# One GpSimd subtraction over a whole tile in place of seven and of four over slices of 256 columns

## The chip, the cores and the metric

The program runs on one core of a Trainium2 chip. Its time is the device time of one execution in microseconds (us); lower is better. The kernel before takes 2143.12 us, the median of 3 runs (2141.82 to 2145.76).

A core has five engines with a queue each, and they meet only at semaphores: TensorE (PE in the profile; its weight loads are PEld), VectorE (DVE), ScalarE (ACT), GpSimd (POOL) and SyncE (SP), which here issues the DMAs. An engine works through its queue in order; an instruction that waits holds up everything behind it on that engine.

## The reference, cut to what matters

Three layers follow each other: windowed attention, a mixture of eight experts with a gating matrix that is normalised eight times over rows and columns, and a feed-forward layer with a leaky activation.

```python
# attention: q, k, v are (4, 8, 576, 64); window 128, a linear bias per head
scores = np.where(mask, scale * q @ k.T + bias, -1e9)
attn = exp(scores - max); attn = attn / (sum(attn) + 1e-9)
x = (attn @ v)                                   # laid out as (2304, 512)

# experts: w1 (8, 512, 1024), w2 (8, 1024, 512)
P = np.exp(x @ w_gate - max)
for _ in range(8):
    P /= P.sum(1, keepdims=True) + 1e-09
    P /= P.sum(0, keepdims=True) + 1e-09
    P *= N / E
for e in range(E):
    out += P[:, e:e+1] * (np.maximum(x @ w1[e], 0.0) @ w2[e])

# feed-forward: w_in (512, 2048), w_out (2048, 512)
h = out @ w_in
return np.maximum(0.01 * h, h) @ w_out
```

## The kernel before, in words

**Stages.** Attention takes the first 175 us or so of the span. Then come 80 "granules": 32 of the experts for the first half of the tokens (numbers 0 to 31), 32 for the second half (32 to 63), 8 of the feed-forward layer for the first half (64 to 71) and 8 for the second (72 to 79). A granule is a slice of 256 hidden columns of one expert or of the feed-forward layer. It has two "units", u = 0 with 256 columns of tokens per operand and u = 1 with 320. Where the half or the layer changes (before granules 32, 64 and 72; a "turn" in what follows), the operands made from x are built anew.

**Weights in two parts.** To keep accuracy each operand of a matmul is held as a high part (the value rounded to the fast float type) and a low part (value minus high part), and each product is three matmuls: high x high, low x high, high x low (lines 1110, 1112 and 1113 up; 1132, 1133 and 1134 down).

**Seven products.** The up-projection of a unit is done as a two-by-two block product with seven products instead of eight. Its operands on the weight side are seven blocks of 256 columns, three raw and four sums. The weights arrive by DMA in `stage_up` (512 KB) and `stage_down` (512 KB). GpSimd makes the blocks and splits them, in `split_up`: four sums of 256 columns (lines 351 to 356), one cast of all 7 x 256 = 1792 columns to `up_hi` (line 358), then the subtraction that gives `up_lo` (line 362). `split_down` does the same for the 1024 columns of the down weights, with a cast (line 368) and a subtraction (line 372). GpSimd's last instruction of each gives the semaphore that TensorE waits for (`up_split`, `down_split`), and that lets SyncE load the next weights.

**When GpSimd works.** There are two sets of split weights. `both(n, s)` (line 436) splits the weights of granule n when TensorE has done the last up product of granule n - 2 (`a_done`), and the down weights when it has done that granule's last down product (`y_done`). So the up split of granule n runs while TensorE is in unit u = 0 of granule n - 1. Two of the 80 splits are made elsewhere: that of granule 0 during attention, and that of granule 1 at its end.

**A unit on the other engines.** TensorE's order in a unit is: two products, a tile of down-projection, two products (the second named A12 and S2 in the code), a tile, the products S4 and S3, a tile, the product A22, one or two tiles. S3 waits for ScalarE's copy `u2` (line 542), A22 waits for VectorE's sum `c22s` (line 863). VectorE's order is: the result of a tile (line 751 or 757), the sum `c11s` (857), the result of a tile, the low part of `c11s` (878), the sums `c22s` (863) and `c12s` (869), a result, the low parts of `c22s`, of `c12s` and of the last block (878), results. In the feed-forward layer the low parts are line 884, and the leaky activation adds in-place operations on `c11s`, `c22s` and `c12s` (887). ScalarE makes the high parts: after the copies of a unit's start it waits for `c11s` (line 593, or 616 in the feed-forward layer), and only then makes the copy `u2`.

The lines that read two operands in SBUF on VectorE are 878 for `c11s` and `c12s` and `c22s` (with `hs_hi`), 884 and 887, and at the turns 834 to 851; lines 857, 863, 869, 751 and 757 have one operand in PSUM.

Of the kernel before, what the change touches and what calls it, by code (L numbers as in the profile page):

```python
# [5 lines left out]
def attention_moe_ffn(nc, q, k, v, w_gate, w_up, w_down, out):  # L6
# [6 lines left out]
    ALU, ACT, AX = mybir.AluOpType, mybir.ActivationFunctionType, mybir.AxisListType  # L13
# [4 lines left out]
    D, E = w_gate.shape  # L18
# [3 lines left out]
    FG = 256  # L22
# [17 lines left out]
    OPS = 7  # L40
# [8 lines left out]
    with ctx:  # L49
# [3 lines left out]
        def place(name, cols, dt=fp32):  # L53
            t = nc.alloc_sbuf_tensor_at(name, [P, cols], dt, offset=at[0])
            at[0] += (cols + 7) // 8 * 32
            return t
# [11 lines left out]
        up_hi, up_lo, down_hi, down_lo, slot_at = [], [], [], [], []  # L68
# [7 lines left out]
        stage_up = place("stage_up", (OPS + 1) * FG)  # L76
        stage_down = place("stage_down", 2 * D)
# [50 lines left out]
        def sem(name):  # L128
            return ctx.enter_context(nc.semaphore(name))
# [19 lines left out]
        up_ready, down_ready, w_step, up_split, down_split = (  # L149
            sem(n) for n in ("up_ready", "down_ready", "w_step", "up_split", "down_split"))  # L150
# [173 lines left out]
        def _(pool):  # L324
            g = nc.gpsimd
# [16 lines left out]
            def raw(op):  # L342
                return stage_up[:, (op + 1) * FG:(op + 2) * FG]
# [3 lines left out]
            def split_up(n, s):  # L347

                pool.wait_ge(up_ready, 16 * (n + 1))
                base = 5 * n  # L350
                g.tensor_tensor(raw(T1), b12, raw(B11), ALU.subtract).then_inc(w_step, 1)  # L351
                g.tensor_tensor(raw(T3), raw(B22), b12, ALU.subtract)
                pool.wait_ge(w_step, base + 1)
                g.tensor_tensor(raw(T2), raw(B22), raw(T1), ALU.subtract).then_inc(w_step, 1)
                pool.wait_ge(w_step, base + 2)
                g.tensor_tensor(raw(T4), raw(B21), raw(T2), ALU.subtract).then_inc(w_step, 1)
                pool.wait_ge(w_step, base + 3)
                g.tensor_copy(up_hi[s][:, :], stage_up[:, FG:]).then_inc(w_step, 1)  # L358
                pool.wait_ge(w_step, base + 4)
                for op in range(OPS):  # L360
                    part = slice(op * FG, (op + 1) * FG)
                    last = g.tensor_tensor(up_lo[s][:, part], raw(op), up_hi[s][:, part], ALU.subtract)  # L362
                last.then_inc(up_split, 1)

            def split_down(n, s):

                pool.wait_ge(down_ready, 16 * (n + 1))
                g.tensor_copy(down_hi[s][:, :], stage_down[:, :]).then_inc(w_step, 1)  # L368
                pool.wait_ge(w_step, 5 * n + 5)
                for c in range(0, 2 * D, FG):  # L370
                    part = slice(c, c + FG)
                    last = g.tensor_tensor(down_lo[s][:, part], stage_down[:, part], down_hi[s][:, part], ALU.subtract)  # L372
                last.then_inc(down_split, 1)

            split_up(0, 0)
            split_down(0, 0)

            def first_operands(u):
# [43 lines left out]

            pool.wait_ge(p_tr, GROUPS * ITERS)
            split_up(1, 1)
            split_down(1, 1)

            def raw_lows(phase, u):
# [8 lines left out]
            def both(n, s):  # L436

                pool.wait_ge(a_done, 4 * 2 * (n - 1))
                split_up(n, s)
                pool.wait_ge(y_done, TILES * (n - 1))  # L440
                split_down(n, s)
# [861 lines left out]
```

## Time and profile before

| | |
|---|---|
| runs, median (lowest to highest) | 2143.12 us (2141.82 to 2145.76) |
| profiled execution, its own time | 2145.76 us |
| profiled execution, span of the core | 2142.8 us |
| TensorE busy | 2094.1 us, 98% of the span |
| VectorE busy | 1299.9 us, 61% |
| GpSimd busy | 1212.8 us, 57% |
| ScalarE busy | 627.7 us, 29% |
| chain of waits, by engine | PE 88%, DVE 9%, issue 3% |
| mean granted TensorE clock | 0.983 of full |

The span is what the instructions of the program cover; the execution's own time is some 3 us more. A busy share near 100% says which engine the others have to feed. The share of an engine that is not the bound counts only where the bound waits for it. The rows further down give a start in us from the span's start, a duration, the engine, the line of the kernel, the operation, what it writes and reads, and the shape.

### The profile page before, as it was taken

The page shows a single profiled execution, that of the slowest core. Times are in us where ns is not written, and L with a number is a line of the kernel's source. Part 1 is how long each engine was busy: PE and PEld are TensorE (multiplying, and loading weights), DVE is VectorE, ACT ScalarE, POOL GpSimd, SP SyncE. Part 2 cuts the span into 40 slices and gives each one's busy share as a digit, 9 for nine tenths or more (in the row PEclk, how much of TensorE's full clock was granted, in tenths as well). Part 3 has the DMA queues.
Part 4 walks back from the last instruction along what each step waited for, and adds up shares of the span by engine and source line. Part 5 has one row for each costly group of instructions (what it writes and reads, how often), then busy time and mean ns, then how long its engine had stood idle before and what let it go on. Part 6 is the DMA issues. An engine that isn't in the chain of part 4 may idle for free.

```text
span 2142.8 us, 37354 instructions
## 1 busy us (share of the span) xinstructions
PE 2094.1 (98%) x12635; PEld 1857.9 (87%) x12635; DVE 1299.9 (61%) x2743; ACT 627.7 (29%) x1712; POOL 1212.8 (57%) x1424
## 2 busy tenths in 40 slices
PE   8989999999999999999999999999999989998999
PEld 5669889999989999988999999999999979997998
DVE  7882775555555555567555555555555586768666
ACT  6863222222222222223222222222222233233222
POOL 3252555655665565567565566556555676667561
PEclk9987999999999999999999999999999999999999
DMA  4431011111111111111111111111111111110211
GB/s 117 92 72 46 30 50 40 39 49 49 39 41 47 49 39 49 49 39 40 40 40 49 49 39 43 47 47 39 49 49 39 39 40 40 50 50 30 94 40 45
DMA packets 83860, 103.66 MB, mean 48 GB/s; under 512 B 61008, under 2 KB 61008, under 8 KB 83792
## 3 DMA queue, kind: packets, MB, share of 16 engines
q1 hardware_dynamic: 83792, 102.80, 14.9%
q8 instruction: 37, 0.61, 0.1%
q14 instruction: 31, 0.25, 0.0%
HBM read 98.06 MB, written 4.72 MB: 48 GB/s over the span
## 4 chain that ended last, share of the span: by engine, by line
PE 88%; DVE 9%; issue 3%; ACT 0%; DMA 0%; SPq 0%; DVEq 0%
PE bank L1132 15%; PE bank L1133 15%; PE bank L1134 15%; PE bank L1110 13%; PE bank L1113 13%; PE bank L1112 13%; DVE sc L704 2%; DVE sc L688 1%; PE bank L1157 1%; PE bank L1057 1%; PE bank L1021 1%; PE bank L1029 1%; DVE hs_lo L878 0%; DVE acc L757 0%; PE bank L1148 0%
## 5 line engine op out<-in xcount | busy, mean ns | idle before, releaser
L757 DVE SCALAR_TENSOR_TENSOR acc<-bank,gate,acc 128x512 f32<-128x512 f32 x540 | 404.4, 749 | 583.5 <-PE bank L1134 583.2
L1110 PE MATMUL bank<-x_hi,up_hi 128*128 128x256 f32 (+1 forms) x2240 | 666.8, 298 | 14.6 <-ACT u L542 13.9
L1113 PE MATMUL bank<-x_hi,up_lo 128*128 128x256 f32 (+1 forms) x2240 | 665.5, 297 | 0.0
L1112 PE MATMUL bank<-x_lo,up_hi 128*128 128x256 f32 (+1 forms) x2240 | 665.0, 297 | 0.0
L1132 PE MATMUL bank<-down_hi,hs_hi 128*128 128x512 f32 x1440 | 569.6, 396 | 7.1 <-DVE acc L757 4.3
L1133 PE MATMUL bank<-down_lo,hs_hi 128*128 128x512 f32 x1440 | 569.2, 395 | 0.0
L1134 PE MATMUL bank<-down_hi,hs_lo 128*128 128x512 f32 x1440 | 561.5, 390 | 0.0
L1110 PEld LDWEIGHTS bank<-x_hi,up_hi 128*128 128x128 f32 x2240 | 426.2, 190 | 44.5 <-ACT u L542 15.9
L1112 PEld LDWEIGHTS bank<-x_lo,up_hi 128*128 128x128 f32 x2240 | 426.3, 190 | 23.6
L1113 PEld LDWEIGHTS bank<-x_hi,up_lo 128*128 128x128 f32 x2240 | 426.4, 190 | 0.0
L362 POOL TENSOR_TENSOR up_lo<-stage_up,up_hi 128x256 fp32r<-128x256 f32 x560 | 420.3, 786 | 6.4
L351 POOL TENSOR_TENSOR stage_up<-stage_up 128x256 f32<-128x256 f32 x80 | 72.0, 900 | 551.2 <-PE bank L1113 497.8
L1134 PEld LDWEIGHTS bank<-down_hi,hs_lo 128*128 128x128 f32 x1440 | 271.6, 189 | 61.9
L1132 PEld LDWEIGHTS bank<-down_hi,hs_hi 128*128 128x128 f32 x1440 | 272.5, 189 | 46.5 <-issue 7.5
L1133 PEld LDWEIGHTS bank<-down_lo,hs_hi 128*128 128x128 f32 x1440 | 272.5, 189 | 32.5
L372 POOL TENSOR_TENSOR down_lo<-stage_down,down_hi 128x256 fp32r<-128x256 f32 x320 | 229.4, 749 | 6.4
L368 POOL CAST down_hi<-stage_down 128x1024 fp32r<-128x1024 f32 x80 | 84.5, 1056 | 228.6 <-PE bank L1134 228.6
L598 ACT ACTIVATE hs_hi<-c22s 128x256 fp32r<-128x256 f32 (+1 forms) x128 | 57.1, 446 | 370.6 <-DVE c22s L863 370.6
L532 ACT ACTIVATE t<-bank 128x256 f32<-128x256 f32 (+1 forms) x160 | 65.4, 409 | 319.2 <-PE bank L1113 318.9
L751 DVE TENSOR_TENSOR acc<-bank,acc 128x512 f32<-128x512 f32 x144 | 98.9, 687 | 93.2 <-PE bank L1134 92.8
L593 ACT ACTIVATE hs_hi<-c11s 128x256 fp32r<-128x256 f32 (+1 forms) x128 | 56.9, 444 | 317.9 <-DVE c11s L857 317.9
L358 POOL CAST up_hi<-stage_up 128x1792 fp32r<-128x1792 f32 x80 | 134.9, 1686 | 5.2
(126 smaller groups left out, 2082.2 us busy)
## 6 DMA issues: line engine op xcount, KB each, us to landing
stage_up<-w_up SPq DMA_DIRECT2D x80, 512.0 KB, 3.2
stage_down<-w_down SPq DMA_DIRECT2D x80, 512.0 KB, 3.2
q_nat<-q SPq DMA_DIRECT2D x32, 128.0 KB, 2.4
k_nat<-k SPq DMA_DIRECT2D x32, 128.0 KB, 2.7
v_nat<-v SPq DMA_DIRECT2D x32, 128.0 KB, 2.3
result<-acc SPq DMA_DIRECT2D x16, 256.0 KB, 2.8
q_nat<-q SPq DMA_DIRECT2D x16, 32.0 KB, 2.3
k_nat<-k SPq DMA_DIRECT2D x16, 32.0 KB, 2.1
```

The lines of the kernel that those rows point to most:

```text
L358: g.tensor_copy(up_hi[s][:, :], stage_up[:, FG:]).then_inc(w_step, 1)
L362: last = g.tensor_tensor(up_lo[s][:, part], raw(op), up_hi[s][:, part], ALU.subtract)
L368: g.tensor_copy(down_hi[s][:, :], stage_down[:, :]).then_inc(w_step, 1)
L372: last = g.tensor_tensor(down_lo[s][:, part], stage_down[:, part], down_hi[s][:, part], ALU.subtract)
L751: last = d.tensor_tensor(to, y[:, :], to, ALU.add)
L757: last = d.scalar_tensor_tensor(out=to, in0=y[:, :], scalar=share(g, tile, e), in1=to, op0=ALU.mult, op1=ALU.add)
L1110: m.matmul(to[:, 0:n], up_hi[s][:, w], x_hi[u][:, x], start=first and c == 0, stop=False, skip_group_check=True)
L1112: m.matmul(to[:, 0:n], up_hi[s][:, w], x_lo[u][:, x], start=False, stop=False, skip_group_check=True)
L1113: last = m.matmul(to[:, 0:n], up_lo[s][:, w], x_hi[u][:, x], start=False, stop=c == 1, skip_group_check=True)
L1132: m.matmul(to[:, :], hs_hi[u][:, h], down_hi[s][:, w], start=f == 0, stop=False)
L1133: m.matmul(to[:, :], hs_hi[u][:, h], down_lo[s][:, w], start=False, stop=False)
L1134: last = m.matmul(to[:, :], hs_lo[u][:, h], down_hi[s][:, w], start=False, stop=f == 1)
```

## The change

In `split_up` the loop of seven subtractions over slices of 256 columns becomes one instruction over 1792 columns, and in `split_down` the loop of four becomes one over 1024 columns. What is computed, the buffers and the semaphores stay.

```diff
@@ split_up
                 g.tensor_copy(up_hi[s][:, :], stage_up[:, FG:]).then_inc(w_step, 1)
                 pool.wait_ge(w_step, base + 4)
-                for op in range(OPS):
-                    part = slice(op * FG, (op + 1) * FG)
-                    last = g.tensor_tensor(up_lo[s][:, part], raw(op), up_hi[s][:, part], ALU.subtract)
-                last.then_inc(up_split, 1)
+                g.tensor_tensor(up_lo[s][:, :], stage_up[:, FG:], up_hi[s][:, :], ALU.subtract).then_inc(up_split, 1)
@@ split_down
                 g.tensor_copy(down_hi[s][:, :], stage_down[:, :]).then_inc(w_step, 1)
                 pool.wait_ge(w_step, 5 * n + 5)
-                for c in range(0, 2 * D, FG):
-                    part = slice(c, c + FG)
-                    last = g.tensor_tensor(down_lo[s][:, part], stage_down[:, part], down_hi[s][:, part], ALU.subtract)
-                last.then_inc(down_split, 1)
+                g.tensor_tensor(down_lo[s][:, :], stage_down[:, :], down_hi[s][:, :], ALU.subtract
+                                ).then_inc(down_split, 1)
```

GpSimd's queue at one split, before (the names' numbers tell the two sets of buffers apart; the last column is what an instruction waits for):

```order
L351 TENSOR_TENSOR stage_up<-stage_up 128x256 [waits up_ready,a_done]
L352 TENSOR_TENSOR stage_up<-stage_up 128x256
L354 TENSOR_TENSOR stage_up<-stage_up 128x256 [waits w_step]
L356 TENSOR_TENSOR stage_up<-stage_up 128x256 [waits w_step]
L358 CAST up_hi_56<-stage_up 128x1792 [waits w_step]
L362 TENSOR_TENSOR up_lo_57<-stage_up,up_hi_56 128x256 [waits w_step]
L362 TENSOR_TENSOR up_lo_57<-stage_up,up_hi_56 128x256 x6
L368 CAST down_hi_58<-stage_down 128x1024 [waits down_ready,y_done]
L372 TENSOR_TENSOR down_lo_59<-stage_down,down_hi_58 128x256 [waits w_step]
L372 TENSOR_TENSOR down_lo_59<-stage_down,down_hi_58 128x256 x3
```

and in the changed kernel, at the same split:

```order
L351 TENSOR_TENSOR stage_up<-stage_up 128x256 [waits up_ready,a_done]
L352 TENSOR_TENSOR stage_up<-stage_up 128x256
L354 TENSOR_TENSOR stage_up<-stage_up 128x256 [waits w_step]
L356 TENSOR_TENSOR stage_up<-stage_up 128x256 [waits w_step]
L358 CAST up_hi_56<-stage_up 128x1792 [waits w_step]
L360 TENSOR_TENSOR up_lo_57<-stage_up,up_hi_56 128x1792 [waits w_step]
L365 CAST down_hi_58<-stage_down 128x1024 [waits down_ready,y_done]
L367 TENSOR_TENSOR down_lo_59<-stage_down,down_hi_58 128x1024 [waits w_step]
```

Nothing is moved past anything else: seven rows and four rows have become one each, the waits stand at the same places, and the queues of the other four engines are the same apart from line numbers, which are 5 lower behind this place.

## Rows read from the trace of the kernel before

**Rows 1.** Waits of all engines: who waited for what, us in total, times, longest.
```profile
POOL stage_up L351 <- PE bank L1113: 497.8, 75, 32.4
...
PE bank L1110 <- ACT u L542: 13.9, 8, 4.3
```

**Rows 2.** Timeline of GpSimd and VectorE at a cast, granule 2: start, us, what.
```profile
249.32 1.82 POOL L358 CAST up_hi<-stage_up 128x1792 fp32r<-128x1792 f32 x1
...
249.53 1.96 DVE L878 SCALAR_TENSOR_TENSOR hs_lo<-c12s,hs_hi 128x320 fp32r<-128x320 f32 x1
251.41 0.48 DVE L878 SCALAR_TENSOR_TENSOR hs_lo<-bank,hs_hi 128x320 fp32r<-128x320 f32 x1
```

**Rows 3.** Line 362, durations min/median/max in ns; a GpSimd group of 640 columns.
```profile
L362 POOL TENSOR_TENSOR up_lo<-stage_up,up_hi x560: 718/741/1381, 25.3 to 2094.5; 128x256 fp32r<-128x256 f32 x187
...
L390 POOL TENSOR_TENSOR sum_a<-x_raw 128x640 f32<-128x640 f32 x1 | 1.5, 1534 | 0.2 <-POOL x_lo L388 0.2
```

**Rows 4.** Timelines by engine, two expert granules: up split, VectorE behind it, product A22.
```profile
1190.67 5.10 POOL L362 TENSOR_TENSOR up_lo<-stage_up,up_hi 128x256 fp32r<-128x256 f32 x7
...
1195.04 0.28 PE L1110 MATMUL bank<-x_hi,up_hi 128*128 128x256 f32 x1
...
1214.15 5.11 POOL L362 TENSOR_TENSOR up_lo<-stage_up,up_hi 128x256 fp32r<-128x256 f32 x7
...
1216.80 0.47 DVE L878 SCALAR_TENSOR_TENSOR hs_lo<-c11s,hs_hi 128x256 fp32r<-128x256 f32 x1
1217.45 0.42 DVE L863 TENSOR_TENSOR c22s<-bank,t 128x256 f32<-128x256 f32 x1 [0.18 <-PE bank L1113]
...
1218.64 0.28 PE L1110 MATMUL bank<-x_hi,up_hi 128*128 128x256 f32 x1
```

**Rows 5.** The same in a feed-forward granule; PE at S3 and A22.
```profile
1842.93 5.75 POOL L362 TENSOR_TENSOR up_lo<-stage_up,up_hi 128x256 fp32r<-128x256 f32 x7
...
1842.92 0.42 DVE L887 SCALAR_TENSOR_TENSOR c11s<-c11s 128x256 f32<-128x256 f32 x1
...
1845.12 0.49 DVE L884 TENSOR_TENSOR hs_lo<-c11s,hs_hi 128x256 fp32r<-128x256 f32 x1
...
1845.02 0.28 PE L1110 MATMUL bank<-x_hi,up_hi 128*128 128x256 f32 x1
...
1847.13 0.28 PE L1110 MATMUL bank<-x_hi,up_hi 128*128 128x256 f32 x1
```

**Rows 6.** Granule 66: first piece of line 362, VectorE, ScalarE, and PE at S3.
```profile
1793.11 0.74 POOL L362 TENSOR_TENSOR up_lo<-stage_up,up_hi 128x256 fp32r<-128x256 f32 x1
...
1793.53 0.59 DVE L887 SCALAR_TENSOR_TENSOR c11s<-c11s 128x256 f32<-128x256 f32 x1
...
1794.48 0.36 ACT L542 ACTIVATE u<-bank 128x256 f32<-128x256 f32 x1
...
1796.08 0.28 PE L1110 MATMUL bank<-x_hi,up_hi 128*128 128x256 f32 x1
```

**Rows 7.** Granule 1, where the gating matrix is normalised on VectorE.
```profile
226.46 5.15 POOL L362 TENSOR_TENSOR up_lo<-stage_up,up_hi 128x256 fp32r<-128x256 f32 x7
...
226.51 0.72 DVE L766 TENSOR_SCALAR row_sum<-row_sum 128x18 f32<-128x18 f32 x1
...
228.09 0.42 DVE L773 TENSOR_REDUCE col_part<-gate 128x8 f32<-128x144 f32 x1
...
228.56 0.39 PE L1163 MATMUL bank<-col_part,ones 128*128 128x8 f32 x2 [0.21 <-DVE col_part L773]
```

**Rows 8.** The turn at granule 32: first piece of line 362, VectorE's sum, PE.
```profile
979.09 1.20 POOL L362 TENSOR_TENSOR up_lo<-stage_up,up_hi 128x256 fp32r<-128x256 f32 x1
...
979.73 1.25 DVE L846 TENSOR_TENSOR sum_b<-x_raw 128x640 f32<-128x640 f32 x1
...
983.83 0.47 PE L1132 MATMUL bank<-down_hi,hs_hi 128*128 128x512 f32 x1 [1.70 <-DVE acc L757]
```

**Rows 9.** GpSimd in attention, the up subtractions of granule 0.
```profile
25.33 5.02 POOL L362 TENSOR_TENSOR up_lo<-stage_up,up_hi 128x256 fp32r<-128x256 f32 x7
```

## The prediction, made before the changed kernel was run

> **What bounds the kernel now.** I read the busy table first: TensorE is busy for 2094.1 of 2142.8 us, so 49 us at most can be gained, and any new wait of TensorE in the 80 granules is paid in full. The second view is who waits for whom [rows 1]. GpSimd waits for TensorE 75 times in 80 splits, 497.8 us in all: the splits are ready long before they are needed. TensorE's largest wait in the granules is for ScalarE's copy u2, 13.9 us in 8 places; no line of TensorE waits for line 362 or 372. So the subtractions are off the path, and what they take or save counts only through somebody else. The third view, the timelines, says through whom.
>
> **What GpSimd does to VectorE.** In [rows 2] GpSimd's cast of 1792 columns runs from 249.32 to 251.14. VectorE starts the low part of c12s at 249.53 and ends at 251.49, 0.35 us behind the cast: 1.96 us for work whose neighbour, with one operand in PSUM, takes 0.48 us while line 362 is running. In [rows 6] VectorE's line 887, 0.59 us, ends at 1794.12, 0.27 us behind the end of the first subtraction (1793.11 + 0.74 = 1793.85). So a VectorE instruction with both operands in SBUF that comes second stands still until the GpSimd instruction has ended, however long that is, and then needs 0.28 us more (256 columns); one with an operand in PSUM is not touched. The order counts, not the number: GpSimd waits likewise when VectorE was first. The Trainium skill says the same (SBUF — State Buffer, section Who interferes with whom): a VectorE instruction with two SBUF inputs and a GpSimd one that reads SBUF exclude each other for the whole instruction. By that rule, and the trace agrees, the seven slices were seven chances for VectorE to get in, and the change leaves one.
>
> **How long the new instruction is.** The trace has none of 1792 columns with two inputs. From the shortest of 256 columns, 718 ns, to 640 columns, 1534 ns [rows 3], a column costs 2.125 ns: 718 + 1536 x 2.125 = 3.98 us. Bounds: not below 1.82 us, the cast of 1792 columns with one input [rows 2]; not above 5.11 us, the seven in a row [rows 4]. I take 3.98, since the slope rests on the same operation. For the down weights it is 718 + 768 x 2.125 = 2.35 us. The Trainium skill (GPSIMD Engine Reference, section Elementwise — side-by-side cycle accounting) gives 4497 ns for 2048 columns; in proportion that is an estimate of 3.93 us, and the sum below would be 4 us less.
>
> What is saved on GpSimd, some 1.1 us a split, is worth nothing: GpSimd idles behind it, and the next weights that SyncE may load sooner are waited for by a GpSimd that waits for TensorE anyway. If that cover were gone, TensorE's waits would name up_lo, and none does.
>
> **The cost, part by part.**
> - *Expert granules.* In the one of 1214.15 [rows 4] the new instruction ends at 1214.15 + 3.98 = 1218.13. VectorE comes to the low part of c11s at 1216.80, now ends at 1217.27, and will end at 1218.13 + 0.28 = 1218.41. Behind it in its queue is c22s: it starts 0.08 us before that end (as in [rows 2], 251.41 against 251.49) and takes 0.42, so 1218.75; TensorE starts 0.05 us after a sum it waits for (228.09 + 0.42 to 228.56, [rows 7]), so 1218.80. The product A22, which needs c22s, starts now at 1218.64: 0.16 us of new wait. The granules come in pairs; in the other one (1190.67, A22 at 1195.04) it is 1190.67 + 3.98 + 0.67 - 1195.04 = 0.28. The mean is 0.22, and 55 granules have this pattern (5 to 31 and 36 to 63): 12.1 us. Each starts afresh, since GpSimd is released by TensorE one unit later and VectorE has caught up by then. Granules 33 to 35 have transposes ahead of A22 and lose nothing.
> - *Feed-forward granules* [rows 5]. VectorE's line 887 is 0.01 us ahead of GpSimd, which therefore begins 0.28 us late (its first slice takes 1.01 us there) and ends at 1842.93 + 0.28 + 3.98 = 1847.19. Line 884 of c11s waits from 1845.12; A22 can start at 1847.19 + 0.67 = 1847.86 instead of 1847.13: 0.73 us, 10 granules (68 to 71, 73 to 78): 7.3 us.
> - *Granules 66 and 67.* Here GpSimd comes 0.42 us ahead of line 887 [rows 6]. Line 887 then ends at 1793.11 + 3.98 + 0.28 = 1797.37, and ScalarE, whose queue has u2 behind the high part of c11s, starts u2 0.36 us after it and takes 0.36, so 1798.09; TensorE's S3 can start at 1798.14 instead of 1796.08: 2.06 us, twice, 4.1 us.
> - *Granules 1 to 4*, with the gating matrix on VectorE [rows 7]. Line 766 (SBUF to SBUF, held 0.72 us now) would be held to 226.46 + 3.98 = 230.44 instead of some 227.15, and the column sum that TensorE waits for hangs on it: 3.3 us less the 0.2 that line 770 loses now. I take 3.1 once and 1.2 for each of the other three, where fewer lines are caught: 6.7 us, between 2 and 12.
> - *The three turns* [rows 8]. GpSimd's first slice there ends at 980.29, having waited for VectorE until about 979.56; line 846 comes at 979.73. It would be held to 979.56 + 3.98 = 983.54, 3.25 us later, and TensorE already waits 1.70 us for the result that stands behind it in VectorE's queue. 3.25 x 3 = 9.8 us. Bounds: 0, if VectorE regains it because nothing holds it later, and 5.6 each, if the down subtraction holds it once more for 2.35.
> - *Attention* [rows 9]. The split of granule 0 falls on VectorE's in-place scaling (line 704), which TensorE waits for now and then. Held up to 3.98 + 2.35 us, less the several short holds it has now: 3 us, between 0 and 6.
>
> The sum is 12.1 + 7.3 + 4.1 + 6.7 + 9.8 + 3.0 = 43.0 us. The profiled execution took 2145.76 us, 2.6 above the median; 2188.8 there is **2186 us** at the median, 2.0% slower. 0.1 us more or less of the new instruction's length is worth 7 us (74 places hang on it: 55, 10, 2, 4 and 3). TensorE's clock I leave as it is: waits of this size stand in [rows 8] in a trace whose mean granted clock is 0.983.
>
> **The rivals.**
> 1. *The feed-forward tie falls the other way.* Line 887 is only 0.01 us ahead of GpSimd [rows 5]. If GpSimd gets there first, those granules become like 66 and 67: u2 is ready at 1842.93 + 3.98 + 0.28 + 0.72 + 0.05 = 1847.96 and S3 was due at 1845.02: 2.94 us instead of 0.73, ten times: 22 us more, 2208 us. Against it: nothing ahead of the tie changes in the queues.
> 2. *Only the special places pay.* If the new instruction takes 3.7 us or less, the expert granules have their cover: c22s is in time, and the feed-forward ones lose 0.45 each. 2143 + 4.5 + 4 + 6 + 9 + 3 = 2169 us. For it: the margin is only 0.16 to 0.28 us; against it: the slope would have to be 9% lower.
> 3. *It gets faster.* At the turns the slices cost GpSimd 1.20 us instead of 0.74 and VectorE 1.25 [rows 8]; they alternate, each stopping the other. With one long hold instead of many short ones, VectorE might spend it on lines with an operand in PSUM and then run free. If that gives back half of the 13.9 us of [rows 1], and the steady granules keep their cover, it is 2136 us. The point from which it decides is a length of 3.25 us: only under that do the feed-forward granules keep A22 in time too (1847.13 - 0.67 - 0.28 - 1842.93).
> 4. *Nothing.* If a long instruction with two inputs let VectorE in between its parts, or the slack were larger than I see, it is 2143 us. Against it stands the cast that held VectorE for its whole 1.8 us [rows 2].
>
> **How the numbers follow.** 0.70 for the forecast (own range 2170 to 2202, from 0.15 us either way in the length and the bounds of the special places), 0.10 for the first rival, 0.09 for the second, 0.06 for the third, 0.05 for the fourth. A difference under 0.2%, 4 us, can't be told from none. Slower: 0.70 + 0.10 + 0.09, and 0.01 of the fourth, 0.90; same 0.05; faster 0.05. The range of 2163 to 2209 leaves out the last two rivals and the outer part of the first.
>
> **What would show it.** Right: one POOL group of 80 with a mean near 4 us; VectorE's low part of c11s at 1.6 to 2.6 us instead of 0.42; a new row "PE L1110 <- DVE c22s" with over 60 waits and some 19 us; two waits of 2 us for u2 in granules 66 and 67; VectorE's busy time 100 us up with the same instructions. Wrong: a length under 3.7 us, or VectorE's rows no longer than now, or TensorE's waits below 60 us in all.

## The result, and the profile after

The changed kernel takes **2211.21 us**, the median of 4 runs (2209.99 to 2212.97); the kernel before, run beside it on the same chip, took 2144.44 us (2141.82 to 2147.75). The ratio is 1.0314, with a 95% interval of 1.0301 to 1.0327. The prediction was 2186 us with a range of 2163 to 2209: slower, as forecast, and for the reason forecast, but 3.1% where 2.0% were expected, and just beyond the end of the range.

The profiled execution took 2211.04 us, its span is 2208.3 us: 65.5 us more than before. The page of the profile (busy time in us, share of the span, number of instructions; then the chain that ended last; then groups of instructions with their busy time, mean in ns and the idle time before them):

```profile
PE 2118.2 (96%) x12635; PEld 1858.5 (84%) x12635; DVE 1399.1 (63%) x2743; ACT 627.8 (28%) x1712; POOL 1084.5 (49%) x704
...
PE 78%; DVE 13%; issue 8%; ACT 0%; DVEq 0%; DMA 0%; SPq 0%; ACTq 0%
...
L360 POOL TENSOR_TENSOR up_lo<-stage_up,up_hi 128x1792 fp32r<-128x1792 f32 x80 | 328.7, 4109 | 6.4
...
L367 POOL TENSOR_TENSOR down_lo<-stage_down,down_hi 128x1024 fp32r<-128x1024 f32 x80 | 193.0, 2413 | 6.4
```

GpSimd does less (1212.8 us before) and VectorE is "busy" for 99 us more with the same 2743 instructions: it stands still inside them. The joined subtraction is 4.109 us in the mean: 4.07 in the steady expert granules, 4.02 in granules 66 and 67, 4.33 to 4.35 in the feed-forward ones, where VectorE is ahead of it and it is held itself; 3.98 was worked out from [rows 3]. The subtraction of the down weights is 2.41 where 2.35 was expected. The same view of the waits as [rows 1], for TensorE and its weight loads:

```profile
PEld bank L1105 <- DVE c22s L858: 47.0, 69, 1.9
...
PE bank L1105 <- ACT u L537: 19.4, 10, 3.6
PE bank L1024 <- DVE sc L699: 19.1, 7, 6.6
PE bank L1105 <- DVE c22s L858: 14.6, 38, 1.5
...
PE bank L1158 <- DVE col_part L768: 8.2, 4, 3.3
```

`c22s` is now waited for in 69 weight loads, 47.0 us; before it was 4 weight loads and 2.3 us (in the rows of the matmuls 0.7 us before, 14.6 now). The span less TensorE's busy time is 48.7 us before and 90.1 after, 41.4 more; the other 24.1 us of the loss lie inside its *busy* time: short waits that the modelled ends of matmuls cover, and stretches at half clock, both read below.

**A steady expert granule**, the counterpart of [rows 4] (start, duration, what):

```profile
1247.19 4.06 POOL L360 TENSOR_TENSOR up_lo<-stage_up,up_hi 128x1792 fp32r<-128x1792 f32 x1
...
1249.83 1.70 DVE L873 SCALAR_TENSOR_TENSOR hs_lo<-c11s,hs_hi 128x256 fp32r<-128x256 f32 x1
1251.45 0.41 DVE L858 TENSOR_TENSOR c22s<-bank,t 128x256 f32<-128x256 f32 x1
...
1251.92 0.19 PEld L1105 LDWEIGHTS bank<-x_hi,up_hi 128*128 128x128 f32 x1 [0.52 <-DVE c22s L858]
...
1251.44 0.39 PE L1129 MATMUL bank<-down_hi,hs_lo 128*128 128x512 f32 x1
1251.92 0.38 PE L1105 MATMUL bank<-x_hi,up_hi 128*128 128x256 f32 x1
1252.14 0.28 PE L1107 MATMUL bank<-x_lo,up_hi 128*128 128x256 f32 x1
```

The subtraction ends at 1251.25, the low part of `c11s`, started at 1249.83, ends 0.28 us behind it at 1251.53, `c22s` ends at 1251.86, and A22 starts at 1251.92. The steps are the predicted ones. Two things are not. The weight load of A22 starts *with* its matmul; before, this row stood 0.23 us ahead of its matmul (1218.64):

```profile
1218.41 0.19 PEld L1110 LDWEIGHTS bank<-x_hi,up_hi 128*128 128x128 f32 x1
...
1218.75 0.28 PE L1112 MATMUL bank<-x_lo,up_hi 128*128 128x256 f32 x1
```

and the first matmul of A22 holds TensorE for 0.22 us (1251.92 to 1252.14) instead of 0.11 (1218.64 to 1218.75). And no idle time is shown in front of A22's matmul: matmul L1129 is drawn 0.39 us long, though in a steady row the next one starts 0.23 us behind it, so 0.16 us of real waiting are covered by its modelled end, and the 0.09 us that are left go unmarked.

**A feed-forward granule** [rows 5], **granule 66** [rows 6] and **granule 1** [rows 7], by engine:

```profile
1916.98 4.33 POOL L360 TENSOR_TENSOR up_lo<-stage_up,up_hi 128x1792 fp32r<-128x1792 f32 x1
...
1916.96 0.42 DVE L882 SCALAR_TENSOR_TENSOR c11s<-c11s 128x256 f32<-128x256 f32 x1
...
1919.16 2.43 DVE L879 TENSOR_TENSOR hs_lo<-c11s,hs_hi 128x256 fp32r<-128x256 f32 x1
...
1921.98 0.39 PE L1105 MATMUL bank<-x_hi,up_hi 128*128 128x256 f32 x1 [0.65 <-DVE c22s L858]
...
1838.21 4.02 POOL L360 TENSOR_TENSOR up_lo<-stage_up,up_hi 128x1792 fp32r<-128x1792 f32 x1
...
1838.64 3.88 DVE L882 SCALAR_TENSOR_TENSOR c11s<-c11s 128x256 f32<-128x256 f32 x1
...
1842.88 0.37 ACT L537 ACTIVATE u<-bank 128x256 f32<-128x256 f32 x1
...
1843.30 0.39 PE L1105 MATMUL bank<-x_hi,up_hi 128*128 128x256 f32 x1 [1.96 <-ACT u L537]
...
231.63 4.01 DVE L761 TENSOR_SCALAR row_sum<-row_sum 128x18 f32<-128x18 f32 x1
...
236.78 0.39 PE L1158 MATMUL bank<-col_part,ones 128*128 128x8 f32 x2 [3.30 <-DVE col_part L768]
```

In the feed-forward granule VectorE is still first, by 0.02 us, so the first rival did not come; in granule 66 GpSimd is first and VectorE stands for 3.88 us. In granule 1 an instruction over 18 columns takes 4.01 us.

**The turn at granule 32** [rows 8]:

```profile
1006.00 4.47 POOL L360 TENSOR_TENSOR up_lo<-stage_up,up_hi 128x1792 fp32r<-128x1792 f32 x1
1010.41 1.23 POOL L365 CAST down_hi<-stage_down 128x1024 fp32r<-128x1024 f32 x1
...
1006.52 4.22 DVE L873 SCALAR_TENSOR_TENSOR hs_lo<-c22s,hs_hi 128x256 fp32r<-128x256 f32 x1
1010.67 1.25 DVE L873 SCALAR_TENSOR_TENSOR hs_lo<-c12s,hs_hi 128x256 fp32r<-128x256 f32 x1
...
1013.01 0.77 PE L1127 MATMUL bank<-down_hi,hs_hi 128*128 128x512 f32 x1 [4.85 <-DVE acc L752]
```

It was the low part of `c22s` that was caught, not the sum that the prediction named (846), and the cast of the down weights caught the next one at once. At the turn at 64 it was the activation of `c12s` (4.20 us), at 72 the sum `sum_a` (4.08 us). TensorE waits 4.85 us instead of 1.70.

**The clock.** In granule 71 the joined subtractions lead to a wait of 2.31 us for `u2`, from 1981.9 to 1984.20. One us later the granted clock falls to half, 1.2 of 2.4 GHz, for some 3.4 us (stretch, its length, PE busy and matmuls, granted clock, DMA):

```profile
1984.20:1985.20 1.00, 1.00 (x7) 1.00 0.00 0
1985.20:1988.60 3.40, 3.40 (x11) 0.50 0.00 0
1988.60:1992.00 3.40, 3.40 (x23) 1.00 0.00 0
```

TensorE is "busy" throughout, but issues 11 matmuls instead of some 20. Behind the 3.30 us in granule 1, behind 1.79 us in granule 2 and behind long waits of the turns at 64 and 72 it does the same.

What an execution loses at half clock varies even where nothing was changed. `fine_turn`, one of the kernels below, is edited at the turns alone and loses 3.2 us more in granule 0; `dose3` leaves the turns alone and loses 2.6 us more at the turn at 64, with 2.1 us less of waiting. The drops in granules 1, 2 and 71 come again in the other kernels with the same waits; how the loss at one turn divides into waiting and clock, one pair of traces does not show.

**Where the 65.5 us are.** Both traces are cut at TensorE's first up product of each granule, and the spacing of its starts is compared pair by pair; growth of single spacings (up to 0.27 us each) where the clock stands at half is counted as clock, the rest as waiting.

| part | predicted | waiting | at half clock |
|---|---|---|---|
| expert granules 5 to 31, 36 to 63 | 12.1 | 23.3 (0.42 each; 0.59 in 31 and 63) | 0 |
| 10 feed-forward granules | 7.3 | 9.1 (0.91 each) | 0 |
| granules 66, 67 | 4.1 | 4.4 | 0 |
| granules 1 to 4 | 6.7 | 7.0 | 2.9 |
| turns in 32, 64, 72 | 9.8 | 6.7 | 4.1 |
| 65, and the rest of 71 | 0 | 1.3 | 1.6 |
| attention | 3.0 | 5.1 in all | |
| sum | 43.0 | 65.5 in all | 8.5 of them |

### The profile page after: what moved, and what is told of

It reads as the page before. It is cut to its first block, busy times and chain, and to the rows that moved or that the text cites. A ratio compares the mean times of both kernels' runs of the same rounds, so it can differ in the third digit from the quotient of the medians.

```text
span 2208.3 us, 36634 instructions
## 1 busy us (share of the span) xinstructions
PE 2118.2 (96%) x12635; PEld 1858.5 (84%) x12635; DVE 1399.1 (63%) x2743; ACT 627.8 (28%) x1712; POOL 1084.5 (49%) x704
## 4 chain that ended last, share of the span: by engine, by line
PE 78%; DVE 13%; issue 8%; ACT 0%; DVEq 0%; DMA 0%; SPq 0%; ACTq 0%
PE bank L1127 13%; PE bank L1128 13%; PE bank L1129 13%; PE bank L1105 12%; PE bank L1108 11%; PE bank L1107 11%; DVE hs_lo L873 2%; DVE sc L699 2%; DVE c22s L858 1%; DVE sc L683 1%; PE bank L1152 1%; DVE hs_lo L879 1%; DVE c11s L882 1%; PE bank L1052 1%; PE bank L1016 1%
## 5 line engine op out<-in xcount | busy, mean ns | idle before, releaser
L1105 PE MATMUL bank<-x_hi,up_hi 128*128 128x256 f32 (+1 forms) x2240 | 674.8, 301 | 36.7 <-ACT u L537 19.4
L1129 PE MATMUL bank<-down_hi,hs_lo 128*128 128x512 f32 x1440 | 563.6, 391 | 0.0
L1105 PEld LDWEIGHTS bank<-x_hi,up_hi 128*128 128x128 f32 x2240 | 427.3, 191 | 92.4 <-DVE c22s L858 47.0
L360 POOL TENSOR_TENSOR up_lo<-stage_up,up_hi 128x1792 fp32r<-128x1792 f32 x80 | 328.7, 4109 | 6.4
L1129 PEld LDWEIGHTS bank<-down_hi,hs_lo 128*128 128x128 f32 x1440 | 272.5, 189 | 62.4
L367 POOL TENSOR_TENSOR down_lo<-stage_down,down_hi 128x1024 fp32r<-128x1024 f32 x80 | 193.0, 2413 | 6.4
```

Source lines behind the costliest of these rows:

```text
L360: g.tensor_tensor(up_lo[s][:, :], stage_up[:, FG:], up_hi[s][:, :], ALU.subtract).then_inc(up_split, 1)
L367: g.tensor_tensor(down_lo[s][:, :], stage_down[:, :], down_hi[s][:, :], ALU.subtract).then_inc(down_split, 1)
L1105: m.matmul(to[:, 0:n], up_hi[s][:, w], x_hi[u][:, x], start=first and c == 0, stop=False, skip_group_check=True)
L1129: last = m.matmul(to[:, :], hs_lo[u][:, h], down_hi[s][:, w], start=False, stop=f == 1)
```

## The experiments

**Which of the two subtractions.** `up_only` joins the seven of the up weights and leaves the down weights in slices; `down_only` is the reverse. The edits undo one half each:

```diff
 up_only, against the changed kernel
-                g.tensor_tensor(down_lo[s][:, :], stage_down[:, :], down_hi[s][:, :], ALU.subtract
-                                ).then_inc(down_split, 1)
+                for c in range(0, 2 * D, FG):
+                    part = slice(c, c + FG)
+                    last = g.tensor_tensor(down_lo[s][:, part], stage_down[:, part], down_hi[s][:, part], ALU.subtract)
+                last.then_inc(down_split, 1)
 down_only, against the changed kernel
-                g.tensor_tensor(up_lo[s][:, :], stage_up[:, FG:], up_hi[s][:, :], ALU.subtract).then_inc(up_split, 1)
+                for op in range(OPS):
+                    part = slice(op * FG, (op + 1) * FG)
+                    last = g.tensor_tensor(up_lo[s][:, part], raw(op), up_hi[s][:, part], ALU.subtract)
+                last.then_inc(up_split, 1)
```

> One subtraction of 1792 columns for the up weights, the four slices of 256 for the down weights as before. If the steady cost comes from the long up subtraction holding VectorE's low part of c11s (the theory), the expert granules stay at 23.96 and 24.09 us and the feed-forward ones at 24.51, and only the special places (attention, granules 1 to 4, turns) gain: 2206 us, between 2200 and 2211. If the down subtraction carries a good part of the steady cost (rival), it is under 2195 us and the expert granules fall below 23.8 us.

> One subtraction of 1024 columns for the down weights, the seven slices for the up weights as before. Theory: no VectorE instruction with two operands in SBUF comes within the 2.4 us of it in a steady granule, so these stay at 23.60 us, and only attention, the gating granules and the turns lose: 2149 us, between 2144 and 2155. Rival (the down part matters as much as the up part): 2165 us or more.

Measured: `up_only` 2208.38 us against 2146.82, ratio 1.0288 (1.0270 to 1.0305); `down_only` 2150.82, ratio 1.0021 (1.0010 to 1.0031). The two add up to the whole (1.0309 against 1.0314). With `up_only` a steady expert granule takes 23.96 or 24.07 us, with `down_only` 23.60 as before. So the 1792 columns make nine tenths of the loss. The largest single place in what the down subtraction adds is granule 71, 2.3 us of some 4. It holds nothing there. It ends 0.4 us sooner than its slices did, and so GpSimd's next instruction, a low part of x for the turn, starts just ahead of VectorE's sum `sum_a` where it used to start just behind it. The rows before, then those of the changed kernel:

```profile
1925.53 4.92 POOL L433 TENSOR_TENSOR x_lo<-xr,x_hi 128x512 fp32r<-128x512 f32 x3
...
1925.34 0.80 DVE L834 TENSOR_TENSOR sum_a<-xr 128x512 f32<-128x512 f32 x1
...
1978.29 4.67 POOL L428 TENSOR_TENSOR x_lo<-xr,x_hi 128x512 fp32r<-128x512 f32 x3
...
1978.52 1.62 DVE L829 TENSOR_TENSOR sum_a<-xr 128x512 f32<-128x512 f32 x1
```

All that stands behind `sum_a` is 0.8 us late, `u2` too. In `down_only` GpSimd is first as well, in `up_only` VectorE is and `sum_a` takes 0.80 us. The same pair shows the clock's share. In `down_only` TensorE's wait is

```profile
1935.10 0.63 PE L1108 MATMUL bank<-x_hi,up_hi 128*128 128x320 f32 x1 [2.32 <-ACT u L540]
```

and the 3.4 us behind it were granted 0.53; in `up_only`

```profile
1984.21 0.41 PE L1107 MATMUL bank<-x_hi,up_hi 128*128 128x320 f32 x1 [1.51 <-ACT u L539]
```

and the 3.4 us behind it 1.00, as before the change. For 0.8 us more of waiting TensorE pays 2.3. The two other kernels below with a joined down subtraction, `low_behind` and `five_two`, have this order and the drop in granule 71 too.

**Is it the hold, or the length of the split?** In `low_behind` the subtraction stays joined, but VectorE's low part of `c11s` stands behind the two sums; in `five_two` VectorE's order stays, and the subtraction is cut into 1280 and 512 columns.

```diff
 low_behind, against the changed kernel (and the same with plain_low in the other unit)
                 sums(k, 1)
-                low(k, u, 1, 0, 0, c11s)
                 sum_22(k, u)
                 sum_12(k, u)
+                low(k, u, 1, 0, 0, c11s)
 five_two, against the changed kernel
-                g.tensor_tensor(up_lo[s][:, :], stage_up[:, FG:], up_hi[s][:, :], ALU.subtract).then_inc(up_split, 1)
+                for p0, p1 in ((0, 5 * FG), (5 * FG, OPS * FG)):
+                    last = g.tensor_tensor(up_lo[s][:, p0:p1], stage_up[:, FG + p0:FG + p1], up_hi[s][:, p0:p1],
+                                           ALU.subtract)
+                last.then_inc(up_split, 1)
```

> The changed kernel with VectorE's low part of c11s moved behind its sums c22s and c12s, in both kinds of unit. GpSimd's instructions are as long as in the changed kernel. Theory (c22s stands in VectorE's queue behind an instruction that is held): A22 finds c22s in time, the steady granules go back to 23.60 us in the experts (53 x 0.42) and in the feed-forward layer (10 x 0.91), about 2178 us, between 2170 and 2187; the low part itself is held for less than 1 us. Rival (a long GpSimd instruction slows TensorE or the split in another way, or up_split comes too late): 2205 us or more and granules of 24 us.

> The changed kernel with the up subtraction in two instructions, 1280 columns and 512. At 2.125 ns a column the first takes 2.9 to 3.0 us. Theory: VectorE comes 2.2 to 2.65 us after the start and is let in at 3.0, c22s is in time in every steady granule, and what the special places lose shrinks with the hold: 2171 us, between 2164 and 2180. Rival (what costs is that slices were joined at all, whatever the length): 2200 us or more.

Measured: `low_behind` 2179.88 us, ratio 1.0155 (1.0138 to 1.0172), half of the loss gone; `five_two` 2172.4 us, ratio 1.0118 (1.0100 to 1.0136). In both the steady granules, expert and feed-forward, are back at 23.60 us. In `low_behind` GpSimd's instruction is as long as ever, and `c22s` no longer knows of it:

```profile
1236.57 4.07 POOL L360 TENSOR_TENSOR up_lo<-stage_up,up_hi 128x1792 fp32r<-128x1792 f32 x1
...
1239.88 0.42 DVE L858 TENSOR_TENSOR c22s<-bank,t 128x256 f32<-128x256 f32 x1 [0.57 <-PE bank L1108]
1240.22 0.42 DVE L864 TENSOR_TENSOR c12s<-bank,u 128x256 f32<-128x256 f32 x1
1240.55 0.41 DVE L873 SCALAR_TENSOR_TENSOR hs_lo<-c11s,hs_hi 128x256 fp32r<-128x256 f32 x1
```

`c22s` has an operand in PSUM and runs from 1239.88 in the midst of the subtraction (to 1240.64). In `five_two` the low part comes while the first piece runs and is let in between the pieces:

```profile
1229.87 4.39 POOL L361 TENSOR_TENSOR up_lo<-stage_up,up_hi 128x1280 fp32r<-128x1280 f32 x2
...
1232.52 0.59 DVE L876 SCALAR_TENSOR_TENSOR hs_lo<-c11s,hs_hi 128x256 fp32r<-128x256 f32 x1
```

So the loss in the 63 steady granules (53 and 10) hangs on one VectorE instruction being caught, not on the time of GpSimd's work. The Trainium skill (SBUF — State Buffer, section Who interferes with whom) has the rule: a VectorE instruction with two SBUF inputs contends with a GpSimd one that reads SBUF, and one with at most one SBUF input does not, outside VectorE's 2-port modes. Both sides of it are seen here: 1.70 us against 0.42. What `low_behind` leaves are the special places: granules 1 to 4 cost 9.5 us, 66 and 67 4.5, granule 71 2.4, the three turns 14.0, of which 6.7 at half clock.

**What a late `c22s` costs TensorE.** `dose3` and `dose5` take the kernel *before* and put three or five short reductions over 144 columns, whose result nobody reads, ahead of the sum `c22s` in unit 0 of the expert granules that run in a loop. GpSimd is left alone; the sum is late by VectorE's own time.

```diff
                 low(k, u, 1, 0, 0, c11s)
+                if u == 0 and not isinstance(k, int):
+                    for to, c in ((esum, 0), (esum_eps, 0), (einv, 0), (neg_max, 0), (esum, E))[:3]:
+                        d.reduce_sum(to[:, c:c + E], gate[:, :].rearrange("p (t e) -> p e t", e=E), AX.X)
                 sum_22(k, u)
```

> The kernel before, all slices kept, with three short reductions over 144 columns (one SBUF operand, result not used) on VectorE ahead of the sum c22s in unit u = 0 of the 52 granules that run in loops. GpSimd has no part in it. c22s comes about 0.8 us later, so that A22 could start 0.05 to 0.1 us after its usual time. Theory (a wait that ends late also lays bare A22's weight load, 0.11 us): these granules grow from 23.60 by 0.1 to 0.2 us more than the shift of A22's start, to 23.75 or 23.85, 52 x 0.2 = 10 us, 2154 us. Rival (the extra 0.11 us of the changed kernel is another effect of the long GpSimd instruction): the granules grow by the shift of A22 alone, 23.65 to 23.70, 2148 us.

> The same with five reductions: c22s some 0.7 us later than with three, A22 shifted by about 0.8 us. Theory: granules of 23.60 + 0.8 + 0.11 = 24.5 us, the 0.11 as large as with three, 52 x 0.9 = 47 us, 2190 us. Rival: 24.4 us and 2185 us; the sizes are told apart in the trace, by the start of A22 against the length of its granule.

Measured: `dose3` 2156.79 us against 2145.36, ratio 1.0046 (1.0031 to 1.0062); `dose5` 2191.1, ratio 1.0204 (1.0188 to 1.0219). From the traces, how much later A22 starts in the granule and how much longer the granule takes (us):

| kernel | A22 later by | granule longer by | difference |
|---|---|---|---|
| dose3, the two of a pair, first half of the tokens | 0.068, 0.187 | 0.173, 0.293 | 0.105, 0.106 |
| dose5 | 0.726, 0.845 | 0.833, 0.947 | 0.107, 0.102 |
| changed kernel | 0.254, 0.379 | 0.360, 0.487 | 0.106, 0.108 |

A wait costs its length and 0.10 to 0.11 us more, from 0.07 to 0.85 us alike. The rows of `dose3`, where A22 is late by 0.19 us, suggest why:

```profile
1226.62 0.49 DVE L863 TENSOR_TENSOR c22s<-bank,t 128x256 f32<-128x256 f32 x1
...
1227.16 0.19 PEld L1113 LDWEIGHTS bank<-x_hi,up_hi 128*128 128x128 f32 x1 [0.37 <-DVE c22s L863]
...
1227.16 0.39 PE L1113 MATMUL bank<-x_hi,up_hi 128*128 128x256 f32 x1
1227.39 0.28 PE L1115 MATMUL bank<-x_lo,up_hi 128*128 128x256 f32 x1
```

The weight load is held with the matmul and starts with it (the next matmul follows 0.23 us behind instead of 0.11), as in the changed kernel. GpSimd has no part in it, so the 0.11 us belongs to TensorE's wait and not to the hold. That it is the weight load which takes them is a reading of these rows; no run sets it apart from another cost of starting again.

**Is the reverse a gain?** If joining costs, cutting other long instructions of GpSimd should gain. `fine_turn` takes the kernel before and halves the low parts at the turns; `fine_cast` cuts the cast of 1792 columns in four; `fine_both` does both.

```diff
 fine_turn, against the kernel before
-                    g.tensor_tensor(operand(x_lo, op, u), of, operand(x_hi, op, u), ALU.subtract
-                                    ).then_inc(x_raw_low, 1)
+                    for h in range(2):
+                        last = g.tensor_tensor(operand(x_lo, op, u)[:, h, :], of[:, h, :],
+                                               operand(x_hi, op, u)[:, h, :], ALU.subtract)
+                    last.then_inc(x_raw_low, 1)
 fine_cast, against the kernel before
-                g.tensor_copy(up_hi[s][:, :], stage_up[:, FG:]).then_inc(w_step, 1)
+                for p0, p1 in ((0, 2 * FG), (2 * FG, 4 * FG), (4 * FG, 6 * FG), (6 * FG, OPS * FG)):
+                    last = g.tensor_copy(up_hi[s][:, p0:p1], stage_up[:, FG + p0:FG + p1])
+                last.then_inc(w_step, 1)
```

> The kernel before with the opposite change at the three turns: GpSimd's low parts of x (line 433, 512 and 640 columns, 18 instructions) in two halves each. Theory: VectorE, which alternates with GpSimd there, is let in after 0.75 to 0.9 us instead of 1.3 to 1.6; its queue is 2 to 3 us earlier at each turn, and TensorE waits for it there: 2138 us, between 2134 and 2142. Rival (GpSimd's low parts are what TensorE waits for, or more instructions cost more than they free): 2144 us or more.

> The kernel before with the up cast alone in four pieces; line 433 as before. Both finer cuts together were 13 us faster, the one of line 433 alone 6 us. If the two add up (holds are cut wherever they stand), the cast alone is worth 6 to 8 us: 2138 us. If the cast helps only where line 433 has been cut too (rival: the two act on the same wait at the turns), it is 2142 us or more.

> The same, and GpSimd's cast of 1792 columns (line 358) in four pieces of 512, 512, 512 and 256 columns, in all splits. Theory: in the steady granules nothing changes, since no VectorE instruction with two SBUF operands comes in the cast; in attention, in granules 2 and 3 and at the turns a hold of up to 1.7 us becomes one of 0.6: 1 to 3 us less than with the turns alone, 2136 us. Rival: three more starts of 0.15 us per split push the up subtraction 0.4 us later and with it VectorE's low part of c11s into another slice, which costs as much as it saves.

Measured: `fine_turn` 2139.6 us, ratio 0.9970 (0.9958 to 0.9982); `fine_cast` 2139.43, ratio 0.9967 (0.9955 to 0.9979); `fine_both` **2132.04** us against 2145.36, ratio 0.9938 (0.9924 to 0.9951), faster than both kernels of this case, and 4 us below what was expected. Its trace has the steady granules at 23.60 us, the turns at 2.9, 3.9 and 3.0 us less (3.0 of it from half-clock stretches behind them that are gone), granules 1 to 4 at 2.1 less, attention at 2.5 less, and granule 0, with more of it at half clock, at 1.6 more. Two of TensorE's waits:

```profile
PE bank L1114 <- ACT u L546: 5.6, 5, 2.3
...
PE bank L1114 <- DVE c22s L867: 3.8, 5, 1.3
```

`u2`, 13.9 us in [rows 1], is down to 5.6. Attention's share of these gains is not shown to be real: it moved by +2.0 us in `dose3` and -1.3 in `fine_turn`, neither of which touches it.

**Two more steps, both misses.** `fine_low` adds the order of `low_behind` to `fine_both`; `fine_low_down` also cuts the cast of the down weights in two.

```diff
 fine_low, against fine_both: low(k, u, 1, 0, 0, c11s) and plain_low(...) behind sum_12, as in low_behind
 fine_low_down, against fine_low
-                g.tensor_copy(down_hi[s][:, :], stage_down[:, :]).then_inc(w_step, 1)
+                for c in range(0, 2 * D, 512):
+                    last = g.tensor_copy(down_hi[s][:, c:c + 512], stage_down[:, c:c + 512])
+                last.then_inc(w_step, 1)
```

> Both finer cuts, and VectorE's low part of c11s behind its sums c22s and c12s. Theory: at the turns TensorE waits 3.8 us for c22s, which then no longer stands behind a held low part; 2 to 3 us less than the finer cuts alone, 2129 us; the steady granules stay at 23.60 us, since nothing waits there. Rival: the wait moves on to the next thing in VectorE's queue (the low parts, the results), and the time is that of the finer cuts, 2132 us.

> The same, and the cast of the down weights in two pieces of 512 columns. It holds VectorE for at most 0.6 us instead of 1.05, at the turns and in granule 1 only: 0 to 1 us less than the one before it; no difference that can be measured is what I expect.

Measured: `fine_low` 2140.94 us, ratio 0.9970 (0.9958 to 0.9982); `fine_low_down` 2138.15, ratio 0.9958 (0.9947 to 0.9970), not to be told from the other. The order that saved 30 us beside one long subtraction loses beside seven short ones: eight of the ten feed-forward granules take 24.11 to 24.14 us instead of 23.60, and granule 73 takes 24.47. The rows of `fine_low`:

```profile
1911.67 0.58 DVE L888 TENSOR_TENSOR hs_lo<-c11s,hs_hi 128x256 fp32r<-128x256 f32 x1
1912.17 0.95 DVE L891 SCALAR_TENSOR_TENSOR c22s<-c22s 128x256 f32<-128x256 f32 x1
1913.05 0.96 DVE L891 SCALAR_TENSOR_TENSOR c12s<-c12s 128x256 f32<-128x256 f32 x1
1913.94 0.68 DVE L755 TENSOR_TENSOR acc<-bank,acc 128x512 f32<-128x512 f32 x1
...
1914.67 0.50 PE L1136 MATMUL bank<-down_hi,hs_hi 128*128 128x512 f32 x1 [0.22 <-DVE acc L755]
```

The moved low part (0.58 us) stands ahead of the two activations now, and both take turns with the slices at 0.95 us; before, the first of them took 0.57. From the start of the sum `c12s` to the result behind them it is 2.60 us (1911.34 to 1913.94) where it was 1.70, and the result is late for TensorE. A place in VectorE's queue is good or bad only beside what GpSimd is doing at that time.

## Why the prediction was right in kind and short in size

**Right.** One held instruction of VectorE, then `c22s`, then A22: every step stands in the rows above, with 0.28 us from release to end, and `low_behind` takes it away. Feed-forward granules, 66 and 67, and the waiting in granules 1 to 4 came within 2, 0.3 and 0.3 us of their terms, and the tie in the feed-forward granules did not turn. That only the special places pay (2169 us) is refuted by 53 steady expert granules at +0.42 us; that it is faster, or nothing, by the result. Of the signs, the group of 80 at 4 us, the low part of `c11s` at 1.70 and 2.43 us, the two waits of 2 us and VectorE's 99 us came as written. The row "PE L1105 <- DVE c22s" did not: 38 waits and 14.6 us, because short waits are hidden under modelled ends. The 69 stand in the row of the weight loads.

**The steps that failed.** The chain from the held instruction to A22 was right; what failed are sizes and two terms put at nothing (1 and 5). The sum was 22.5 us short:

1. *"TensorE's clock I leave as it is."* This term was put at nothing. The argument was that waits of 1.70 us stood in a trace with a mean granted clock of 0.983 [rows 8]; but that trace also had three half-clock stretches behind waits of the turns, and waits of 1.8 to 5.6 us were to come. In this pair of traces it cost 8.5 us: 4.5 in granules 1, 2 and 71, which come again in the other kernels with these waits, and some 4 at the turns at 64 and 72, which a single pair leaves unsure. A mean over the span shows it only coarsely, since 0.001 of it is 2 us: it went from 0.983 to 0.979 here, and over the runs of record from 0.982-0.987 (34 runs) to 0.974-0.982 (21 runs).
2. *"TensorE starts 0.05 us after a sum it waits for", and that was all.* The start was right (0.06 us in the rows); that a matmul which has waited holds TensorE 0.11 us longer, with its weight load held too, was left out. 0.11 us in each of 67 granules (55, 10 and 2) is 7.4 us, by the two `dose` kernels.
3. *The length of 3.98 us.* It is 3.97 in attention, but 4.07 in the steady expert granules: 0.09 us more in 67 granules, 6 us (a little less, since 66 and 67 have 4.02). The median slice in place of the shortest would have made it worse: 741 ns and 1536 columns at (1534 - 741) / 384 ns are 3.91 us, an estimate from [rows 3]. The Trainium skill's 4497 ns for 2048 columns (GPSIMD Engine Reference, section Elementwise), by proportion an estimate of 3.93 us, errs the same way. Why it is longer there is open.
4. *The turns, 3.25 us each.* Waiting grew by 4.3, 0.5 and 2.0 us, 3.1 us less than thought; another instruction than the one named was caught at each of them. With the clock they come to 10.8 us, near the 9.8 predicted, and for that a coincidence.
5. *"What is saved on GpSimd, some 1.1 us a split, is worth nothing: GpSimd idles behind it."* The down subtraction, too, had a price at the turns alone. In granule 71 GpSimd does not idle: low parts of x follow that subtraction. The 0.4 us saved there put GpSimd ahead of VectorE's `sum_a`, and cost 0.8 us of waiting and 1.6 of clock. This one is a missing mechanism and not a size.
6. *Attention, 3 us* and 5.1 measured, within its bounds of 0 to 6. The five kernels with a joined subtraction have 2.2 to 5.3 us here and the three that leave attention alone -1.3 to +2.0, so a loss is likely and its size open.

8.5 + 7.4 + 6.0 - 3.1 + 0.8 + 2.1 and 0.8 in granules 31, 63 and 65 make the 22.5.

The prediction's own range for its mechanism ended at 2202 us. It had varied the length and the special places, and held the cost of a wait at exactly its length.

**Open.** What makes the clock fall behind one wait and not another: it did behind 1.79 us in granule 2 and 2.31 in 71, and not behind 1.96 in 66 or 2.50 at the turn at 32; a wait of 1.54 us in granule 1 stands in the kernel before, in the changed one and in `down_only`, and the clock fell behind it in `down_only` alone of the three; in `up_only` granule 67 had it behind a wait of 1.95 us for `u2`, and the same granule of the changed kernel, with the same wait, had none. No run was made on this alone.

## What to carry to other kernels

Before joining instructions of GpSimd, look for VectorE instructions with two SBUF operands that start while they run: each cut is a chance for VectorE to get in, and the engine that does less (GpSimd, 128 us less here) can make the one that bounds the kernel wait. Look also at what follows the shortened instruction: an engine that gets there sooner can take a turn that the other had. Price a new wait of TensorE at its length, plus 0.11 us for starting again, plus, behind the longer ones (1.5 to 5.6 us here, and not behind each), a possible stretch at half clock, and read new waits in the rows of the weight loads, since those of the matmuls hide the short ones. What was coarse in the same way elsewhere (the cast, the low parts at the turns) is then worth cutting: it gave 0.6% on a kernel that seemed to have 49 us to gain at all.

## What the runs showed of the hardware

- A wait on a semaphore that stands before a matmul holds its weight load too. A load that runs 0.23 us ahead otherwise then starts with its matmul, and the wait costs 0.10 to 0.11 us beyond the shift, the same for shifts from 0.07 to 0.85 us.
- Around the wait of 2.3 us in granule 71 the granted clock fell to half (0.50) 1.0 us behind its end in the changed kernel and 1.2 in `low_behind`, and 0.2 and 0.1 us before its end in `down_only` and `five_two`. The cost stands in rows that look busy, matmuls of 512 columns 0.43 us apart instead of 0.23.
- An instruction of VectorE over 18 columns is held as long as any other: line 761 (766 before) takes 4.01 us behind the joined subtraction, 0.72 beside the slices. The reciprocal of the same 18 columns took 0.27 us beside the slices. Line 761 reads one tile in SBUF, so more than the lines with two operands are exposed.
- The same GpSimd instruction takes 3.97 us in attention, 4.02 in granules 66 and 67 and 4.07 in the steady expert granules. Why is open.
